# Splitting weights ahead of a shared PSUM read, and a new timetable for the side work of the first four chunks

## What is computed

```python
# 1: softmax over 7 taps per head, then a causal convolution along the tokens
out = np.einsum('hk,bskhg->bshg', w, x_unf)
# 2: token mixing of a rotated copy, residual, channel mixing
theta = x @ w_theta
zr, zi = x * np.cos(theta), x * np.sin(theta)
y = np.einsum('ts,bsd->btd', w_tok_r, zr) + np.einsum('ts,bsd->btd', w_tok_i, zi)
u = x + y
u + np.maximum(u @ w_ch, 0.0)
# 3: low-rank token mixing, then a two-layer MLP with residual
h = xt @ U @ V
u = x + h.transpose(0, 2, 1)
u + np.maximum(u @ w_ch1, 0.0) @ w_ch2
```

## Time and profile before

| | us |
|---|---|
| median of 3 runs | 2816.72 (2813.64 to 2820.9) |
| the profiled execution | 2817.73 |
| its span, first to last instruction | 2815.7 |

### The profile page before, as it was taken

One profiled execution on the slowest core, in us unless ns is written; L12 is line 12 of the kernel. 1 busy time (PEld: TensorE's weight loads), 2 busy tenths in 40 slices (PEclk: granted clock), 3 DMA queues, 4 the chain that ended last, 5 costly groups with the idle time before them and its releaser, 6 DMA issues.

```text
span 2815.7 us, 37106 instructions
## 1 busy us (share of the span) xinstructions
PE 2754.7 (98%) x14519; PEld 2656.6 (94%) x14519; DVE 2141.1 (76%) x2473; ACT 1035.8 (37%) x1392; POOL 195.6 (7%) x228
## 2 busy tenths in 40 slices
PE   8899889999999999999999999999999999999999
PEld 7899879999999999999999999999999989999999
DVE  6787758878888789788788887987767875656665
ACT  6443233333333333333333333333322443333433
POOL 0101000101101001010010010010100000000000
PEclk9999999999999999999999999999999999999999
DMA  6768547758668667677586686775872000100000
GB/s 203 166 168 185 141 140 187 181 164 202 160 192 188 155 192 182 166 187 182 168 215 150 192 184 165 194 168 161 203 162 80 34 3 20 38 27 29 27 29 34
DMA packets 102349, 396.09 MB, mean 141 GB/s; under 512 B 10656, under 2 KB 28736, under 8 KB 102080
## 3 DMA queue, kind: packets, MB, share of 16 engines
q0 software_dynamic: 31680, 143.29, 29.4%
q1 hardware_dynamic: 70528, 250.83, 25.4%
HBM read 355.15 MB, written 38.93 MB: 140 GB/s over the span
## 4 chain that ended last, share of the span: by engine, by line
PE 93%; DVE 5%; issue 2%; ACT 1%; DMA 0%; DVEq 0%; SPq 0%; ACTq 0%
PE bank L1238 22%; PE bank L1239 22%; PE bank L1237 22%; PE bank L1329 2%; PE bank L1181 2%; PE bank L1332 2%; PE bank L1331 2%; PE bank L1333 2%; PE bank L1330 2%; PE bank L1317 1%; PE bank L1314 1%; PE bank L1316 1%; PE bank L1318 1%; PE bank L1315 1%; DVE attn L837 1%
## 5 line engine op out<-in xcount | busy, mean ns | idle before, releaser
L1237 PE MATMUL bank<-w_h,z_op 128*128 128x424 f32 (+1 forms) x3465 | 1237.2, 357 | 9.0 <-ACT Y L582 5.7
L1238 PE MATMUL bank<-w_l,z_op 128*128 128x424 f32 (+1 forms) x3465 | 1232.2, 356 | 0.0
L1239 PE MATMUL bank<-w_h,z_op 128*128 128x424 f32 (+1 forms) x3465 | 1231.2, 355 | 0.0
L569 ACT ACTIVATE w_h<-w_raw 128x1272 fp32r<-128x1272 f32 x385 | 487.2, 1265 | 1069.6 <-PE bank L1239 972.4
L1237 PEld LDWEIGHTS bank<-w_h,z_op 128*128 128x128 f32 x3465 | 653.9, 189 | 29.1 <-issue 7.4
L1238 PEld LDWEIGHTS bank<-w_l,z_op 128*128 128x128 f32 x3465 | 653.6, 189 | 17.3
L1239 PEld LDWEIGHTS bank<-w_h,z_op 128*128 128x128 f32 x3465 | 652.9, 188 | 16.1
L908 DVE TENSOR_TENSOR w_l<-w_raw,w_h 128x1272 fp32r<-128x1272 f32 x385 | 568.6, 1477 | 79.4 <-ACT w_h L569 79.4
L545 POOL DMA_DIRECT2D w_raw<-in_w_tok x220 | 193.1, 934 | 1927.4 <-DVE w_l L908 1355.1
L1116 DVE SCALAR_TENSOR_TENSOR hid_l<-bank,hid_h 128x384 fp32r<-128x384 f32 x264 | 144.3, 556 | 149.6 <-ACT hid_h L780 147.0
L944 DVE TENSOR_TENSOR Y<-Y,bank 128x1272 f32<-128x1272 f32 (+1 forms) x105 | 154.5, 1472 | 129.9 <-PE bank L1239 129.6
(11 more groups left out here) (127 smaller groups left out, 2963.6 us busy)
## 6 DMA issues: line engine op xcount, KB each, us to landing
w_raw<-in_w_tok SPq DMA_DIRECT2D x220, 636.0 KB, 4.3
w_raw<-in_w_tok POOLq DMA_DIRECT2D x220, 636.0 KB, 6.4
z_raw<-z_out SPq DMA_DIRECT2D x85, 576.0 KB, 6.6
z_out<-zf SPq DMA_DIRECT2D x65, 384.0 KB, 6.5
x_win<-in_xin SPq DMA_DIRECT2D x22, 585.0 KB, 7.1
out<-res SPq DMA_DIRECT2D x22, 576.0 KB, 2.8
v_raw<-in_v SPq DMA_DIRECT2D x11, 144.0 KB, 2.6
w_raw<-in_w SPq DMA_DIRECT2D x1, 1536.0 KB, 6.8
```

Of the source, the lines that this page charges most:

```text
L569: nc.scalar.activation(w_h[:, s % WRING], w_raw[:, SLOT[s]], ACT.Copy).then_inc(wh_ready, 1)
L1237: mm(to, zh, wh, start=(k == 0 and not goes_on), stop=False, skip_group_check=goes_on)
L1238: mm(to, zh, wl, start=False, stop=False, skip_group_check=goes_on)
L1239: last = mm(to, zl, wh, start=False, stop=(k == KC - 1), skip_group_check=goes_on)
```

## The change

Nothing is computed differently. The change has two parts.

**Order in ACT's block.** Where touch belongs to a q = 0 stage (*shared* in the diff), it now comes after w_hi(s+2) instead of ahead of it.

**Another timetable.** The convolution of group 2 starts four blocks earlier (6 instead of 10) and is done in block 12 instead of 15; that of group 3 is done in block 25 instead of 26; groups 5, 6 and 7 go two, three and four blocks later. Phase sets of group 2 move two stages up, those of groups 4 to 7 down, and further apart: for group 4 ahead of stages 39, 43 and 47 instead of 38, 41 and 44, for group 5 ahead of 55, 58 and 61 instead of 52, 55 and 58, for group 6 at 70, 75, 79 instead of 67, 72, 76, for group 7 at 88, 91, 94 instead of 84, 89, 93. EARLY becomes a list: groups 5 and 7 now also have their sines and products ahead of the weight splits. Group 2's residual moves from block 16 to 15. For chunk 2, the loads, additions and splits of the operands of q = 1 to 4 come one to three blocks later.

```diff
@@ -126,30 +126,31 @@
 
 def conv_stage(n, k):
     if n in (1, 2, 3):
-        return {1: (0, 0, 1, 1, 2, 2, 2), 2: (10, 11, 12, 13, 13, 14, 15), 3: (20, 21, 22, 23, 24, 25, 26)}[n][k]
-    return {4: 31, 5: 45}.get(n, PER * (n // 2 - 1) - 11 + 17 * (n % 2)) + k
-
-
-
-EARLY = 4
+        return {1: (0, 0, 1, 1, 2, 2, 2), 2: (6, 7, 8, 9, 10, 11, 12), 3: (19, 20, 21, 22, 23, 24, 25)}[n][k]
+    return {4: 31, 5: 47, 6: 62, 7: 80}.get(n, PER * (n // 2 - 1) - 11 + 17 * (n % 2)) + k
+
+
+
+EARLY = (1, 2, 3, 5, 7)
 
 
 def theta_stage(n, r):
-    if n < 6:
-        return {1: (4, 6, 8), 2: (16, 18, 20), 3: (27, 29, 31), 4: (38, 41, 44), 5: (52, 55, 58)}[n][r]
+    if n < 8:
+        return {1: (4, 6, 8), 2: (14, 16, 18), 3: (27, 29, 31), 4: (39, 43, 47), 5: (55, 58, 61), 6: (70, 75, 79),
+                7: (88, 91, 94)}[n][r]
     return conv_stage(n, 0) + (8, 13, 17)[r]
 
 
 def angle_stage(n, r):
-    return theta_stage(n, r) + (0 if n < EARLY else 1)
+    return theta_stage(n, r) + (0 if n in EARLY else 1)
 
 
 def product_stage(n, r):
-    return theta_stage(n, r) + (1 if n < EARLY else 3)
+    return theta_stage(n, r) + (1 if n in EARLY else 3)
 
 
 def residual_stage(n):
-    return {0: 5, 1: 12}.get(n) or conv_stage(n, TAPS - 1) + 1
+    return {0: 5, 1: 12, 2: 15}.get(n) or conv_stage(n, TAPS - 1) + 1
 
 
 def group_pair(n):
@@ -175,6 +176,8 @@
         return {2: 4, 3: 11, 4: 15, 5: 19, 6: 19}
     if c == 1:
         return {0: -11, 1: -11, 2: -1, 3: 2, 4: 6, 5: 10, 6: 10, 7: 15}
+    if c == 2:
+        return {0: -11, 1: -11, 2: -6, 3: -3, 4: 1, 5: 5, 6: 5, 7: 15}
     return {0: -11, 1: -11, 2: -8, 3: -5, 4: 0, 5: 4, 6: 4, 7: 15}
 
 
@@ -183,6 +186,8 @@
         return {1: 10, 3: 17, 4: 21}
     if c == 1:
         return {0: -9, 1: 1, 3: 8, 4: 12}
+    if c == 2:
+        return {0: -9, 1: -4, 3: 3, 4: 7}
     return {0: -9, 1: -6, 3: 2, 4: 6}
 
 
@@ -191,6 +196,8 @@
         return {1: 12, 2: 14, 3: 18, 4: 23}
     if c == 1:
         return {0: -8, 1: 2, 2: 4, 3: 9, 4: 14, 5: 16, 6: 19}
+    if c == 2:
+        return {0: -8, 1: -2, 2: 0, 3: 4, 4: 14, 5: 16, 6: 19}
     return {0: -8, 1: -5, 2: -1, 3: 3, 4: 14, 5: 16, 6: 19}
 
 
@@ -660,14 +667,18 @@
                 piece_hi(1, r)
 
             for s in range(NS):
-                if s >= 1 and TOUCHES[s - 1] > (TOUCHES[s - 2] if s > 1 else 0):
+                first = s >= 1 and TOUCHES[s - 1] > (TOUCHES[s - 2] if s > 1 else 0)
+                shared = s >= 1 and STAGES[s - 1][1] == 0
+                if first and not shared:
                     touch(s - 1)
-                for n in range(1, EARLY):
+                for n in EARLY:
                     for r in range(KC):
                         if product_stage(n, r) == s:
                             sin(KC * n + r)
                 if s + 2 < NS:
                     w_hi(s + 2)
+                if first and shared:
+                    touch(s - 1)
                 for c in range(CHUNKS):
                     for q, when in z_splits(c).items():
                         if PER * c + when == s:
@@ -679,7 +690,7 @@
                     for r in range(KC):
                         if theta_stage(n, r) == s:
                             turn(KC * n + r)
-                        if n >= EARLY and angle_stage(n, r) == s:
+                        if n not in EARLY and angle_stage(n, r) == s:
                             sin(KC * n + r)
                 if s == PER * (CHUNKS - 1) + 4:
                     act.wait_ge(tail_loaded, 16)
@@ -1008,7 +1019,7 @@
                     for r in range(KC):
                         if angle_stage(n, r) == s:
                             angles(KC * n + r)
-                        if n >= EARLY and product_stage(n, r) == s:
+                        if n not in EARLY and product_stage(n, r) == s:
                             products(KC * n + r)
                 if s >= 1 and STAGES[s - 1][:2] == (CHUNKS - 1, 5):
                     recombine(s - 1, STAGES[s - 1][2])
```

## The result

| | before | changed |
|---|---|---|
| median of 4 runs, us | 2815.53 (2813.64 to 2820.90) | 2765.94 (2764.64 to 2767.24) |
| the profiled execution | 2817.73 | 2767.24 |
| its span | 2815.7 | 2765.2 |

The ratio is 0.9821, 95% interval 0.9804 to 0.9838. Of all the executions behind this text one, of the kernel with the sums held back, took 4537.85 us at a granted clock of 0.57, and no time given here counts it.

The account below looks back on a forecast made before the run. PE was taken as the bound (98% busy, 93% of the chain of waits). Gains 16.3 + 36.2 - 0.9 = 51.6 took the profiled 2817.7 to 2766.1; the median lies 1.0 lower, so 2765 us, range 2758 to 2785.

Parts of the forecast that it names:

- What is lost, 57.4 us: PE's losses in stages 12 to 20 (15.8), 21 to 26 (2.5) and 37 to 60 (39.1): the most reordering can bring.
- The 1.52 us of a phase set: Price of a set on PE: a steady stage takes 5.21 us, one with a phase set 6.73.
- Part 1, touch: Blocks 11 to 14: with touch behind w_hi, DVE gets back 8.5 us of idle time.
- Part 2, front: Stages 12 to 26: group 2's earlier convolution gains 16.3 us, with a new stall of 1.8 ahead of stage 12.
- Part 3, sets of groups 4 and 5: Stages 37 to 60: moved phase sets and products gain 36.2 us, from 39.1 lost less 2.6 and 0.3.
- The wait at 38: PE waits 2.6 us ahead of stage 38 for its operand's split in block 37, formerly hidden under the convolution wait.
- Clock: Slow clock after the two remaining stalls, 1.8 and 2.6 us: costs between 0 and 1.8, taken as 0.9.
- Part 4: Groups 6 and 7 and chunk 2's operands: PE lost nothing from 430 us on, so gain 0.
- The sum: Total gain over the kernel: 16.3 + 36.2 - 0.9 = 51.6 us.
- The front that gets too full: Rival, 0.14: later starts of blocks 11 or 12 reach PE; 2773, or up to 2785 with later dense blocks late.
- Sines in front: Rival, 0.07: sines ahead of weight splits in groups 5 and 7 hold the splits up; about 2790.
- Slower by the sums: Rival, 0.04: POOL's accumulating transfers become the bound, deciding from a landing of 7.7 us; a landing of 12 gives 2834.

Follow-up runs that it names:

- the kernel with the sums held back: Changed kernel, but POOL starts the sum for a stage two after its first weight only after DVE's next evacuation, up to stage 60: 2779.1 us, ratio 0.9870.
- the last experiment: Changed kernel with group 2's tap 4 in block 8, all early groups' sines and products in front, three taps of group 4's convolution moved: 2762.0 us.
- late groups alone: Kernel before with only the new timetable of groups 4 to 7 and of chunk 2's operands: 2783.0 us, ratio 0.9880.
- tap 4 in block 8: Changed kernel with tap 4 of group 2's convolution in block 8 instead of 9: 2765.8 us, ratio 0.9819.
- the split in block 36: Changed kernel with load, addition and split of operand (1, 1) one block earlier, the split in block 36 instead of 37: 2767.2 us, ratio 0.9822.
- all sines in front: Changed kernel with sines and products of groups 4 and 6 also ahead of the weight splits, as for 5 and 7: 2765.2 us, ratio 0.9821.
- sums apart: Changed kernel with group 2's tap 4 in block 8, operand (1, 1) one block earlier, POOL's sums for stages 36 and 37 put off: 2765.9 us.
- both early: Changed kernel with group 2's tap 4 in block 8 and operand (1, 1)'s load, addition and split one block earlier: 2764.8 us, ratio 0.9814.
- the old touch order: Changed kernel with touch ahead of w_hi again everywhere: 2772.9 us, ratio 0.9843.

## Why the prediction was right, point by point

- **What is lost, 57.4 us.** Right but for one price, which made it some 1.4 too large. The 1.52 us of a phase set come from a stage of 6.73 with one of 5.19 behind it; behind most sets the next stage is slower too. Of the changed kernel stages 42, 43, 101 and 102, with sets ahead of 43 and 102:

```profile
core 0: us, PE busy (x) PEld busy (x), PEclk, DMA share, GB/s
267.53:274.31 6.78, 3.37 (x10) 1.69 (x9) 1.00 0.72 211
274.31:279.62 5.31, 3.03 (x9) 1.69 (x9) 1.00 0.93 197
592.45:599.18 6.73, 3.35 (x10) 1.69 (x9) 1.00 1.03 304
599.18:604.37 5.19, 2.99 (x9) 1.69 (x9) 1.00 0.66 169
```

  Where PE does not wait now, stages 12 to 20 take 51.94 for a predicted 51.5, and 21 to 26 take 32.53 for 32.5. In the kernel of the last experiment, where 0.79 us of waiting is left in stages 37 to 60, they take 135.49, so 134.7 for a predicted 133.7.
- **Part 1, touch.** Right in mechanism. DVE's waits for w_h between 90 and 123 us, in blocks 11 to 14, came to this in the kernel before (total, times, longest), for a predicted 8.5:

```profile
DVE w_l L908 <- ACT w_h L569: 8.6, 4, 2.5
```

  With the change this is left, between 115 and 135 us:

```profile
DVE w_l L919 <- ACT w_h L576: 0.6, 1, 0.6
```

  Between 86 and 115 us, where the w_lo of blocks 11 to 14 stand, there is none. What the prediction did not have is a wait of 1.0 us for z_hi in block 14, which ACT does behind the touch. What the order is worth in time, the prediction did not say apart from part 2.
- **Part 2, front.** 16.3 forecast (its terms, 13.9 and 2.5, make 16.4); from the start of stage 1 to that of stage 27 it is 164.32 before and 148.46 now, 15.9. Stage 21 began at 147.73 for "near 149", with a start 1.7 us earlier, so from stage 1 on it was 0.5 later than forecast; most of that is the price of three sets. The wait that it creates is there, 1.56 for 1.8, and was the touch.
- **Part 3, sets of groups 4 and 5.** 36.2 before the clock; 33.8 measured. The wait at 38 is 2.37 for 2.6, and stage 46 with set (4, 2) took 7.11 instead of 6.73, the 0.3 of the forecast. No wait for zf is left over 1 us. Of the 2.4 missing 1.7 is the clock and about 0.9 the price of six sets, with 0.2 back from the shorter wait. Stage 61 began at 374.60 for "near 374"; that is luck in part, since stage 1 began 1.7 us earlier than before.
- **Clock.** The other mis-sized term. The forecast took 0.9, half way between a slow window and none. One came, right behind the wait of 2.37, and stage 38 with the phase set behind it took 8.40 us at 0.80:

```profile
core 0: us, PE busy (x) PEld busy (x), PEclk, DMA share, GB/s
243.39:251.79 8.40, 3.85 (x9) 2.17 (x9) 0.80 0.61 90
95.79:101.10 5.31, 3.05 (x9) 1.69 (x9) 1.00 0.96 219
```

  8.40 less 6.73 is 1.67. This is the profiled execution, the slowest of the four; the others were not traced. After the 1.56 us ahead of stage 12 none came (5.31, 1.00), as the forecast said. The Trainium skill (TensorE: Matmul & The Clock Gate, HAM oscillation) describes a PE that waits for transfers between its bursts and starts each one cold. Carried over to both stalls, as the prediction did for comparison, this holds for the longer one only, and in other kernels of this case not even for that (last section); the measurement decides.
- **Part 4.** 0 forecast. From stage 61 to stage 95 it is 186.72 before, 186.62 now.
- **The sum.** 51.6 forecast, 49.6 between the medians, 49.7 in the stage window. The gain was forecast 2 us too large: 1.4 by the price of a set, 0.8 by the clock, less 0.2 by the wait ahead of stage 38. That 2765 met 2765.9 all the same is luck: the median it started from (2816.7) lay 1.2 above that of all four runs of before.
- **The rivals.** The front that gets too full did not happen: 15.9 of the 16.3 came. Sines in front: no price. Slower by the sums: not there. With the transfers held by 3.8 us it costs 13 us where its own pricing gives 40; the landing of 12 us by which it came to 2834 was not run.

## What to carry to other kernels

Price the ideal of each stretch from its own steady stages; the difference to what it took is the ceiling of any reordering, and here all of it but the 1.4 us of a price too low was waits with a name and the slow clock behind them. Take such a price from several places and not from the cheapest. A step on one engine that waits for another should stand behind what that other engine needs next; and a producer that shares a buffer should be a whole block ahead of its consumer, since at equal places the consumer waits until that block is through (4.0 to 5.3 us each for the four waits for zf here). When a wait is left, take load off the engine that is late before asking for its inputs sooner: here the first gave 1.6 us, and the second moved the wait to another stage.

## What the runs showed of the hardware

- Whether the clock falls after a wait of some 2.4 us is not fixed. Ahead of stage 37 or 38 the changed kernel, the old touch order, late groups alone, tap 4 in block 8 and sums held waited 2.37 us each, the split in block 36 waited 2.29, and all six got a slow window (1.7 us lost in 8.40 at 0.80 granted in the changed kernel). The kernel with all sines in front waited the same 2.37 us, with sums apart 2.44, with both early 2.43, and none of these got one: stage 38 with its set took 6.84 us in the first. Nor did one follow the 2.44 us ahead of stage 16 with the old touch order. A lone wait of 1.8 us or less was never followed by one, and the waits of 2.7 us or more all were. Each kernel was traced once, so whether it is the kernel or the execution that decides is open.
- A store of 384 KB took 11.5 to 12.9 us to land beside POOL's accumulating transfers of 636 KB, at a DMA share of 1.04 to 1.05, against 6.5 in the median; in the changed kernel, where nothing had been asked for earlier, 11.8.
